# Delta-rule attention and two FFNs in one core's program: where the second chunk's lane stages, the triangle loads and the third tile's inverses stand in the queues

## The reference

```python
for t in range(S):                       # k_n is k / (norm(k) + 1e-6)
    y[:, :, t] = einsum('bhd,bhde->bhe', q[:, :, t], state)
    v_old = einsum('bhde,bhd->bhe', state, k_n[:, :, t])
    state = state + beta_t * einsum('bhd,bhe->bhde', k_n[:, :, t], v[:, :, t] - v_old)
```

## Time and profile before

| | us |
|---|---|
| runs | 1023.75, 1025.45, 1025.74 |
| the profiled execution's own time | 1023.27 |
| its span | 1021.3 |
| TensorE busy | 986.1 (97%) |
| VectorE busy | 413.2 (40%) |
| ScalarE busy | 308.5 (30%) |
| GpSimd busy | 218.0 (21%) |

### The profile page before, as it was taken

How to read it: one execution, slowest core, us unless ns; L and a number is a source line. 1 busy time by engine, 2 the same in 40 slices (tenths; PEclk the granted TensorE clock), 3 DMA queues, 4 the chain that set the end, 5 groups by cost and what they waited for, 6 DMA issues and landing times.

```text
span 1021.3 us, 25029 instructions
## 1 busy us (share of the span) xinstructions
PE 986.1 (97%) x11096; PEld 817.6 (80%) x11096; DVE 413.2 (40%) x672; ACT 308.5 (30%) x603; POOL 218.0 (21%) x380
## 2 busy tenths in 40 slices
PE   6589899999999999999999999999999999999998
PEld 5488898778778788778888888888888888888887
DVE  5577555544643644543366322322322322223222
ACT  2255334333333432332355312211212212112211
POOL 2697580760581184000000000000000000000000
PEclk9699999999999999999999999999999999999999
DMA  7767649346246334420162100100100100100000
GB/s 232 190 202 187 167 123 224 100 135 161 85 111 163 101 87 134 107 68 23 44 235 93 63 1 1 62 1 1 62 1 1 62 1 0 63 1 1 31 1 31
DMA packets 120843, 85.60 MB, mean 84 GB/s; under 512 B 94432, under 2 KB 99936, under 8 KB 120736
## 3 DMA queue, kind: packets, MB, share of 16 engines
q1 hardware_dynamic: 110592, 76.07, 26.4%
q10 hardware_dynamic: 10144, 7.93, 2.7%
HBM read 63.28 MB, written 20.71 MB: 82 GB/s over the span
## 4 chain that ended last, share of the span: by engine, by line
PE 89%; DVE 3%; DMA 3%; SPq 2%; issue 1%; ACT 1%; ACTq 0%; DVEq 0%
PE bank L1297 89%; DVE h_lo L1256 1%; DMA tri<-tri_scratch 1%; SPq L644 1%; DMA k_sq<-in_ky 1%; DMA k_dim<-in_kt 0%; DMA tri_scratch<-gram 0%; SPq L655 0%; ACT h_hi L976 0%; DVE norm L1140 0%; ACT gram L1004 0%; DMA gram<-flip_scratch 0%; DVE v_tok L1147 0%; ACT stage L1074 0%; SPq L739 0%
## 5 line engine op out<-in xcount | busy, mean ns | idle before, releaser
L1297 PE MATMUL bank<-x_hi,w_hi 128*128 128x512 f32 (+1 forms) x768 | 293.0, 382 | 1.3 <-DVE x_lo L1231 1.3
L1297 PE MATMUL bank<-x_lo,w_hi 128*128 128x512 f32 (+1 forms) x768 | 288.8, 376 | 0.0
L1297 PE MATMUL bank<-x_hi,w_lo 128*128 128x512 f32 (+1 forms) x768 | 288.7, 376 | 0.0
L1297 PE MATMUL bank<-h_hi,w_hi 128*128 128x512 f32 (+1 forms) x552 | 211.2, 383 | 3.4 <-DVE h_lo L1256 2.9
L1297 PE MATMUL bank<-h_hi,w_lo 128*128 128x512 f32 (+1 forms) x552 | 204.7, 371 | 1.5 <-issue 1.5
L1297 PE MATMUL bank<-h_lo,w_hi 128*128 128x512 f32 (+1 forms) x552 | 204.9, 371 | 0.0
L1276 DVE TENSOR_TENSOR stage<-bank,stage 128x512 f32<-128x512 f32 x72 | 49.8, 692 | 318.5 <-ACT stage L1102 318.5
L1297 PEld LDWEIGHTS bank<-x_hi,w_hi 128*128 128x128 f32 x768 | 144.4, 188 | 29.2 <-DVE x_lo L1231 1.5
L1297 PEld LDWEIGHTS bank<-x_hi,w_lo 128*128 128x128 f32 x768 | 144.5, 188 | 26.4
L1297 PEld LDWEIGHTS bank<-x_lo,w_hi 128*128 128x128 f32 x768 | 144.6, 188 | 25.3
L1250 DVE TENSOR_TENSOR stage<-stage,bank 128x512 f32<-128x512 f32 (+1 forms) x112 | 68.4, 611 | 186.6 <-ACT stage L1074 186.5
(11 more groups left out here) (133 smaller groups left out, 600.8 us busy)
## 6 DMA issues: line engine op xcount, KB each, us to landing
w_raw<-in_w SPq DMA_DIRECT2D x12, 576.0 KB, 3.8
k_dim<-in_kt SPq DMA_DIRECT2D x12, 512.0 KB, 4.4
q_dim<-in_qt SPq DMA_DIRECT2D x12, 512.0 KB, 3.6
x1s<-in_w ACTq DMA_DIRECT2D x14, 384.0 KB, 3.8
k_sq<-in_ky SPq DMA_DIRECT2D x12, 384.0 KB, 3.5
v_tok<-in_vy SPq DMA_DIRECT2D x12, 384.0 KB, 3.2
x_in<-x_scratch SPq DMA_DIRECT2D x6, 768.0 KB, 4.7
out<-out_sb SPq DMA_DIRECT2D x18, 256.0 KB, 2.3
```

What stands on the lines that cost most here:

```text
L1297: return pe.matmul(dst, lhsT, rhs, start=start, stop=stop, **kw)
```

## The change

Four things are moved; no instruction is added or taken away. In ACT_FIRST and DVE_FIRST the stages `("lane", 1)` and `("triangles", 1)` go from behind L 0 and U 0 to behind DZ 0; the weight splits `w1`, the key squares `sq` and the issues `tri 3`, `inv 0`, `fetch` change places around them. In SyncE's list the first `load_q` and the second `load_small` go ahead of `load_ky(0)` and `load_v(0)`, `load_triangles(1)` goes ahead of `load_ky(1)` and `load_k(1)`, and `load_inverses(2)` goes ahead of `load_prep(8)` and `store_both(7)`. In unit 0 the stages `lane 2` and `triangles 2` go from slot 29 to slot 28 (ahead of `h_hi` and `h_lo` of f = 13 and not behind them). In unit 1 the stage G 7 goes from slot 24 to slot 26.

```diff
--- before.py
+++ after.py
@@ -265,14 +265,14 @@
                        ("U", 0): (1, 2), ("Z", 0): (3, 4), ("DZ", 0): (1, 2), ("Y", 0): (7, 0), ("DS", 0): (3, 4),
                        ("X", 0, 0): (1,), ("X", 0, 1): (2,)}
         ACT_FIRST = [("G", 0), ("quarters", 0), ("small lane", 0), ("G", 1), ("quarters", 1), ("G", 2), ("G", 3),
-                     ("fetch", 1), ("fetch", 2), ("sq", 0), ("small lane", 1), ("w1", 0), ("w1", 1), ("tri", 3),
-                     ("inv", 0), ("root", 0), ("fetch", 3), ("fetch", 4), ("E", 0), ("w1", 2), ("L", 0), ("lane", 1),
-                     ("U", 0), ("w1", 3), ("Z", 0), ("w1", 4), ("sq", 1), ("DZ", 0), ("back", 1), ("Y", 0),
+                     ("fetch", 1), ("fetch", 2), ("small lane", 1), ("tri", 3), ("sq", 0), ("w1", 0), ("inv", 0),
+                     ("root", 0), ("w1", 1), ("E", 0), ("fetch", 3), ("fetch", 4), ("L", 0), ("w1", 2), ("U", 0),
+                     ("w1", 3), ("Z", 0), ("w1", 4), ("sq", 1), ("DZ", 0), ("lane", 1), ("back", 1), ("Y", 0),
                      ("fetch", 5), ("fetch", 6), ("X", 0, 0), ("X", 0, 1)]
         DVE_FIRST = [("G", 0), ("norms", 0), ("G", 1), ("small lane", 0), ("S", 0), ("G", 2), ("G", 3), ("solve", 0),
                      ("small lane", 1), ("root", 0), ("S", 1), ("w1", 0), ("scale", 0), ("E", 0), ("w1", 1), ("L", 0),
-                     ("QK", 0), ("U", 0), ("lane", 1), ("Z", 0), ("triangles", 1), ("w1", 2), ("DZ", 0), ("w1", 3),
-                     ("w1", 4), ("Y", 0), ("DS", 0), ("X", 0, 0), ("X", 0, 1)]
+                     ("QK", 0), ("U", 0), ("w1", 2), ("Z", 0), ("w1", 3), ("DZ", 0), ("lane", 1), ("triangles", 1),
+                     ("Y", 0), ("w1", 4), ("X", 0, 0), ("X", 0, 1), ("DS", 0)]
 
         IDLE = 6
 
@@ -318,8 +318,8 @@
                 put(25, "scale", 2)
                 put(26, "KS", 2)
                 put(28, "N1", 1)
-                put(29, "lane", 2)
-                put(29, "triangles", 2)
+                put(28, "lane", 2)
+                put(28, "triangles", 2)
                 put(31, "N2", 1)
             elif u == 1:
                 put(1, "U", 2)
@@ -335,7 +335,7 @@
                 put(18, "Y", 3)
                 put(22, "DS", 3)
                 put(23, "scale", 4)
-                put(24, "G", 7)
+                put(26, "G", 7)
                 for kc in range(KC):
                     put(31 + 2 * (kc > 0), "X", 1, kc)
             else:
@@ -799,18 +799,18 @@
             store_quarters(sp, 0, (0, 1))
             load_small(0)
             store_quarters(sp, 1, (0, 1))
+            load_q(0)
+            load_small(1)
             load_ky(0)
             load_v(0)
-            load_q(0)
-            load_small(1)
             store_small(0)
             load_back(sp, 0, (0, 1))
             load_quarters(sp, 0, (0, 1))
             store_both(2)
             load_ktok(0)
+            load_triangles(1)
             load_ky(1)
             load_k(1)
-            load_triangles(1)
             load_prep(4)
             load_v(1)
             store_small(1)
@@ -850,9 +850,9 @@
             load_ky(5)
             load_ktok(4)
             load_x(3)
+            load_inverses(2)
             load_prep(8)
             store_both(7)
-            load_inverses(2)
             load_triangles(3)
 
             for u in range(2, NIT):
```

## The result

The changed kernel takes 1030.98 us, the median of 4 runs (1029.87 to 1034.61); the kernel before takes 1024.75 us beside it (4 runs). The ratio is 1.0069, 95% interval 1.0047 to 1.0091: some 7 us slower. The prediction said 1023.7 us with a range up to 1026.8 us. It was wrong in sign and outside its range. "Slower" had 0.13. Two runs far above all others (1226.94 us of the version with slot 29 back, 2193.39 us of the kernel before) are counted in no ratio.

A forecast was written before the change was run, and what follows sets the result against it. TensorE, busy 986.1 of 1021.3 us, was taken as the bound, leaving 35.2 us of standstill. Unit 0's 1.6 us plus unit 1's 0.1 us gave 1.7 us less: 1025.45 us becomes 1023.7 us, range 1020.7 to 1026.8 us.

The forecast's parts named there:

- Part 1 (a): First part: with lane 1 behind DZ 0, Z waits only for U's copies and starts 4.6 us earlier.
- Part 1 (b): First part: ScalarE's small-inverse loads follow sooner, so L 0 gains 1.5 us (bounds 0 and 1.7).
- part 2: Solve of tile 1: arrives 2.8 us earlier (bounds 0.2 and 3.6), so N1 moves 3.5 us, to 101.9 us.
- Part 1 (c): First part: `back 1` waits for second small inverses, Y copied at 46.5 to 47.5 us; FFN starts 4 us earlier.
- Part 3: Unit 0: slot 28 makes TensorE wait 2.4 us for `h_lo`, costs 1.9 us; unit 0 ends 1.6 us earlier.
- Part 4: End of unit 1: waits go, 2.2 us, but tile 3's triangles land later; some 0.1 us remain.
- rival D: Unit 2: stalled cross loads delay tile 3's triangles to 181 us or later, holding lane 3; 1027.7 us, 13%.
- B: Solve and unit 2: solve arrives 3.6 us earlier, tile 3's triangles land in time; 1021.2 us, 22%.
- C: First part: solve hardly moves (0.2 to 1 us), ScalarE's stages wait for their loads; about 1025.4 us, 20%.

The follow-up runs named there:

- Lists with SyncE's first part: Kernel before with the new ScalarE and VectorE stage lists and SyncE's new first-part order, nothing else: 1026.26 us, ratio 1.0022.
- the late order: Kernel before with only load_inverses(2) moved ahead of load_prep(8) and store_both(7): 1027.12 us, ratio 1.0028.
- The stage list experiment: Kernel before with only ScalarE's and VectorE's first-part lists (ACT_FIRST, DVE_FIRST) changed: 1025.85 us, ratio 1.0019.
- the SyncE experiment: Kernel before with only SyncE's order of the first part changed: 1025.34 us, ratio 1.0005.
- the late half: Kernel before with G 7 in slot 26 and load_prep(8) moved behind load_triangles(3) in SyncE's order: 1023.8 us, ratio 1.0005.
- the second mixed run: Repeat: kernel before with lane 1 between Z and DZ, `back 1` behind Y, G 7 in slot 26, load_prep(8) behind load_triangles(3): 1024.43 us, ratio 0.9991.

## Why the prediction was wrong

The costs add up. Lists with SyncE's first part 2.2, slot 28 2.4, the late order 2.8, G 7 -0.6 thousandths make 6.8; the whole change has 6.9. Each has about 1.7 to either side, so this bears the decomposition but does not prove that nothing interacts. Taken out of the whole, slot 28 gives back 2.7 and the late order 3.0, nearly what each costs alone; these differences are not much beyond their intervals either. In us the front costs 2.3, slot 28 2.5, and the late order with G 7 2.3 (2.9 less 0.6). The prediction had them at -3.5, +1.9 and -0.1. So of the 8.8 us between the forecast 1.7 us less and the measured 7.1 us more, 5.8 us are the front, 2.4 us the end of unit 1, and 0.6 us slot 28.

**Part 1 (a) held.** Z came 4.9 us closer to U (2.72 us against 7.61), forecast 4.6.

**Part 1 (b) failed, and part 2 with it.** It said that U starts 1.5 us earlier. U started at 37.09 us, 1.1 us later. Two terms were wrong. First, the prediction let ScalarE's four loads start when SyncE's do, at 25.56 us, and left that time where it was. But both wait for the store of the small inverses, and it came later: SyncE's start at 26.94 us, ScalarE's at 26.96 us, 0.3 us sooner than before and not 1.7 us. In all five traces that have both front edits the two engines start within 0.02 us of each other, at 26.02 to 26.96 us. The bound of 0 was right, but its reason was not the one that bound: the square of the keys waited 1.92 us, was done at 25.87 us, and the loads stood for the store after it. In the new order 768 KB of keys and values are asked for 3 us ahead of this store, in the old one 7 us ahead. That they delay it is not shown separately. Second, E 0 and L 0 took 1.99 and 1.98 us, at half clock by their durations, and 1.16 us each in the kernel before. E 0 started 0.2 us earlier, and L 0, which no longer waits for the transposed inverses, waited 0.4 us less. The two slow stages cost 1.65 us, more than the 1.1 us by which U is late. The prediction has no term for the clock, and the edit that moved the queries ahead comes with the slow stretch in all six traces that have it. In the other traces with the new first part U starts at 35.54 to 37.05 us, never near 34.5 us.

Part 2 follows from U. The prediction's own distances put the solve's start at 51.35 us less what DZ gains, so it moves ahead of 47.03 us only if DZ gains more than 4.3 us. The new order ties the solve to DZ's copies; in the kernel before it hung on Z's. The prediction gave DZ the same 6.1 us as Z. Z came 3.8 us earlier and DZ's copies 3.5 us (44.42 against 47.93 us), so the solve started at 47.71 us and not at 45.25 us. The stage list experiment shows this alone: FFN early, solve late, a wait at N1. In all fourteen traces N1 comes 57 to 61 us after the solve's start. Where TensorE waits for the blocks at N1, an earlier FFN buys nothing that the solve doesn't; in the changed kernel's own trace N1 does not wait, and is late for the late FFN start and its matmuls at half clock. N1 "before 101 us or after 104 us" was named as the sign of a wrong prediction; it was 107.72. That the front gains nothing is shown. That it costs 2.3 us is shown by the ratio (interval 0.6 to 3.9 us), and where it loses them is not: on average N1 comes at the same time in the two groups of traces, within 0.1 us.

A part of part 2 did hold. Of the three long instructions at the solve's start one is left:

```profile
48.13 1.05 POOL L544 TENSOR_TENSOR prod<-tri,tinv 128x31 f32<-128x31 f32 x1 [0.17 <-POOL tinv L540]
```

```profile
48.13 0.95 DVE L1235 TENSOR_TENSOR w_lo<-w_spare,w_hi 128x768 fp32r<-128x768 f32 x1
```

They start together, and the 31-element product, 0.24 us in the kernel before without a split beside it, ends 0.1 us after the split. The Trainium skill (page "SBUF — State Buffer", section "Who interferes with whom") calls the port pair of these two engines an exclusive lock; this row agrees. The prediction added that by this rule only the GpSimd instruction is delayed; the section says that the order of issue decides who waits. Here it was the GpSimd instruction, and the split kept its usual 0.95 us.

**Part 1 (c) failed.** I let the second small inverses arrive at 44.5 to 45.5 us "behind the same megabytes of loads". They were not the same: the wait for the triangle stores, which I had moved up in SyncE's queue, bunched 1.8 MB right ahead of them. They were there at 48.9 us, `back 1` issued for 2.85 us and not 1.95 us, and Y was copied at 52.12 us, forecast 46.5 to 47.5. The other traces with this order have them at 46.4 to 49.2 us, all later than forecast, and the three with the same first part copy Y at 48.65 to 50.07 us. I had asked what a moved load goes past and not what comes to wait behind it. The Trainium skill (page "DMA: Bandwidth & Descriptors", section "Queues, rings and completion order") says that each DMA engine takes a queue's descriptors in ring order. The 8.0 us of this small store behind 1.8 MB, and 6.8 us in the SyncE experiment, fit that. But the same edit alone costs nothing that can be told, and letting Y pass `back 1` makes no difference that can be told. So this is a real wait, and is not shown to cost time.

**Part 3 was right in its cost and blind to what stood behind it.** N1 to the last down projection: forecast 10.2 us, measured 10.19 us twice, 10.22 us once, and 11.39 us where the clock fell ahead of it (SyncE's late order undone); the wait for `h_lo`: forecast 2.4, measured 1.92. Missed was the low clock at the end of unit 0. With slot 28 it fell between 111 and 126 us in all four traces. But with slot 29 it fell there too in five of ten (SyncE's first part alone, G 7 alone, both front edits, the late half, and the second mixed run), and stayed at 1.00 in the other five, among them the kernel before and the changed kernel with slot 29 back. So the slot isn't the only way to it, and a pair of traces doesn't show what it adds. By the ratio slot 28 costs 2.5 us, some 0.6 us above the forecast 1.9, which is within the interval.

**Part 4 had the right mechanism and the wrong size, and it was rival D.** The waits of G 7 and N1 went. But I let the triangles be asked for 17.0 us after the flipped inverses are stored; it was 20.4 us. The cross loads took 6.2 us (1.62 and 4.57 us), above the upper bound of 5.9, and the stores with their landing 6.4 us (178.44 to 184.80). This was no accident of one trace: the four traces with this order have 6.2 to 6.5 us for the cross loads and 19.0 to 20.4 us in all. The prediction had named both the price and the threshold: from 1.7 us later on it loses. Rival D with 1.8 us was the mechanism, given 13%, because I took one stalled issue in the trace for an accident. The wait of ScalarE at lane 3 is there in the changed kernel and in the late order alone, 5.79 and 5.71 us, and only 1.58 us in the trace with slot 29 back. In the changed kernel one stalled issue of 3 us is again part of it (in the 4.57 us).

**The rivals.** B fell with (b). C's outcome, a solve that hardly moves, is what happened in the first part, but its reason, ScalarE waiting for the keys of chunk 1, did not bind in the changed kernel's trace: that wait was 0.44 us and over before DZ's matmuls ended. In the trace with slot 29 back it did (2.65 us, and TensorE 2.22 us behind it). D's mechanism happened in unit 2, and its 1027.7 us are still 3 us short of the result. I had set them up as alternatives, each with a chance of its own, where they lie in different parts of the kernel and can both come true. That is also a reason why the range was too narrow.

**Open.** Where the front loses its 2.3 us, and why TensorE's `issue` stalls last up to 3.3 us (7.8 us in all, before 3.6), was not settled. Nor was how much of the 7 us the low clock makes up, as no experiment held it fixed: SyncE's first part alone has the early slow stretch too, and its time can't be told from the kernel before.

## What to carry to other kernels

Before counting a removed wait as gain, follow the second chain to its meeting point (here the solve to N1) and price the edit on that chain first: whichever of the two arrives last sets the time. When a transfer that waits is moved up in an in-order queue, list what now stands behind its wait and what leaves in one burst when it ends. Rivals in different parts of a kernel add up; give each part its own bounds and sum them for the range.

## What the runs showed of the hardware

In the changed kernel's trace TensorE stood still for 1.92 and 0.84 us (`h_lo`) and 3.26 us (`issue`) within 11 us, and then ran at a granted clock of 0.50, 1.2 GHz, until 126 us, which cost 1.5 us more in 16 matmuls. The record of the granted clock can miss a slow stretch: from 55.6 to 61.4 us it reads 1.00 while the matmuls come 0.21 us apart, as they do at 0.50 elsewhere and not at 0.12 us. And issuing is not a fixed price: the four loads of `back 1` on ScalarE's queue took 1.97 us in the kernel before, 2.85 us in the changed kernel, and between 1.83 and 2.96 us over the traces where they were issued in one go, with SyncE's burst ahead of them (1.85 to 2.96 us) and without it (1.83 to 2.11 us). Four cross loads on SyncE's took 2.23 us before and 4.57 us after.
